# Turning the normalised rows of a Trainium2 kernel by transfers and VectorE instead of TensorE

## The reference

```python
# A1: attention of 8 heads of 64, in chunks of 32 queries with 56 keys around them and 8 memory keys
scores = scale * np.matmul(q_c, k_full.transpose(0, 1, 3, 2))
a = softmax(scores);  out[:, :, c_start:c_end] = np.matmul(a, v_full)
# A2: a layer with SoLU and a layer norm over its 1024 hidden values
h = x @ w_in                                   # 512 -> 1024
solu = h * sm                                  # sm = softmax of h over the row
ln = (solu - mu) / np.sqrt(var + 1e-06) * g_ln
x = ln @ w_out                                 # 1024 -> 512
# C: each token goes to one of 8 experts (argmax of x @ w_gate)
h = np.maximum(x[mask] @ w1[e], 0.0);  out[mask] = gate_w * eom * (h @ w2[e])
```

## Time and profile before

| | |
|---|---|
| three runs | 747.57, 749.77, 752.82 us (median 749.77) |
| profiled execution | 749.5 us, its span 747.8 us |
| busy in the span | TensorE 715.8 us (96%), VectorE 474.1 (63%), ScalarE 303.9 (41%), GpSimd 188.9 (25%) |
| mean granted clock of TensorE | 0.991 |
| stage A | to about 385 us |
| transposes of `u_sb` on TensorE | 192 in 24 blocks |

### The profile page before, as it was taken

The page is one execution under the profiler, slowest core; times in us unless marked ns, Lnnn a source line. Parts: engine busy times, 40 slices in busy tenths (PEclk is TensorE's granted clock), DMA queues, the critical chain, the costliest instruction groups (busy, mean ns, idle before and its releaser), DMA issues.

```text
span 747.8 us, 16177 instructions
## 1 busy us (share of the span) xinstructions
PE 715.8 (96%) x5272; PEld 619.3 (83%) x5273; DVE 474.1 (63%) x777; ACT 303.9 (41%) x467; POOL 188.9 (25%) x352
## 2 busy tenths in 40 slices
PE   3899999999999999999989999999999999999985
PEld 2698999899989998999988777888888888888874
DVE  5677788778867676767854647434757556675332
ACT  3543444444443444344423446224444445363220
POOL 3121444434311112111220222221222321321211
PEclk9999999999999999999999999999999999999998
DMA  9713333443232222322013676833969696933220
GB/s 326 258 42 123 107 100 113 144 138 99 71 117 95 71 71 90 122 71 71 30 44 128 225 229 179 225 79 80 243 151 285 169 253 160 237 76 99 63 67 32
DMA packets 43949, 98.70 MB, mean 132 GB/s; under 512 B 6286, under 2 KB 19982, under 8 KB 43792
## 3 DMA queue, kind: packets, MB, share of 16 engines
q1 hardware_dynamic: 22128, 64.82, 27.7%
q10 hardware_dynamic: 15840, 16.52, 9.8%
q0 software_dynamic: 5952, 16.98, 7.2%
HBM read 73.78 MB, written 14.09 MB: 118 GB/s over the span
## 4 chain that ended last, share of the span: by engine, by line
PE 91%; DMA 3%; DVE 3%; issue 2%; ACT 1%; ACTq 1%; POOLq 0%; SPq 0%; POOL 0%; DVEq 0%
PE banks L1213 76%; PE banks L1244 4%; PE banks L1234 3%; PE banks L1266 3%; PE banks L1226 3%; PE banks L1346 2%; DMA r_quads<-r_sb 1%; DMA q_sb<-q_t 1%; DMA xs<-x_rows,rows_now 1%; ACTq L723 1%; DVE he L890 0%; DVE prob L875 0%; PE banks L1369 0%; PE banks L1296 0%; ACT xsT_hi L694 0%
## 5 line engine op out<-in xcount | busy, mean ns | idle before, releaser
L1213 PE MATMUL banks<-slots_hi_lo,rT_hi 128*128 128x512 f32 x464 | 147.3, 399 | 1.9 <-DVE rT_lo L1054 1.9
L1213 PE MATMUL banks<-slots_hi_lo,xsT_hi 128*128 128x512 f32 x464 | 125.9, 394 | 2.8 <-DVE xsT_lo L1043 2.8
L1213 PEld LDWEIGHTS banks<-slots_hi_lo,xsT_hi 128*128 128x128 f32 x464 | 87.4, 189 | 21.8 <-issue 3.9
L1213 PEld LDWEIGHTS banks<-slots_hi_lo,rT_hi 128*128 128x128 f32 x464 | 85.8, 190 | 18.9 <-issue 2.3
L1213 PE MATMUL banks<-slots_hi_lo,rT_lo 128*128 128x512 f32 x232 | 91.5, 394 | 0.0
L1213 PE MATMUL banks<-wout_hi,uT_hi 128*128 128x264 f32 x384 | 83.4, 299 | 2.0 <-DVE uT_lo L879 2.0
L1213 PE MATMUL banks<-wout_hi,uT_lo 128*128 128x264 f32 x384 | 78.7, 287 | 0.0
L1213 PE MATMUL banks<-wout_lo,uT_hi 128*128 128x264 f32 x384 | 78.5, 286 | 0.0
L1043 DVE TENSOR_TENSOR xsT_lo<-banks,xsT_hi 128x512 fp32r<-128x512 f32 x30 | 20.6, 688 | 83.2 <-ACT xsT_hi L694 83.2
L1054 DVE TENSOR_TENSOR rT_lo<-banks,rT_hi 128x1024 fp32r<-128x1024 f32 x29 | 35.5, 1224 | 59.5 <-ACT rT_hi L734 58.0
L1213 PE MATMUL banks<-slots_hi_lo,xsT_lo 128*128 128x512 f32 x232 | 72.2, 393 | 0.0
(11 more groups left out here) (168 smaller groups left out, 1189.9 us busy)
## 6 DMA issues: line engine op xcount, KB each, us to landing
raw_w<-experts SPq DMA_DIRECT2D x56, 512.0 KB, 4.8
r_quads<-r_sb ACTq DMA_DIRECT2D x104, 128.0 KB, 3.7
v_sb<-v_win SPq DMA_DIRECT2D x24, 384.0 KB, 4.6
k_sb<-k_win SPq DMA_DIRECT2D x22, 384.0 KB, 3.5
x_rows<-x SPq DMA_DIRECT2D x24, 264.0 KB, 2.1
q_sb<-q_t SPq DMA_DIRECT2D x24, 256.0 KB, 2.7
stage<-experts POOLq DMA_DIRECT2D x8, 512.0 KB, 5.8
weights<-w_both ACTq DMA_DIRECT2D x4, 512.0 KB, 9.6
```

The source lines that it names most:

```text
L1213: ins = mm(o, lhs, rhs(part, k, n), start=(k == first and lhs is not None and part == 0 and parts == (0, 1)), stop=(k == final and parts = ...
```

## The change

`u_turn` stays on TensorE for blocks 0 and 23. For blocks 1 to 22 SyncE issues four transfers of `u_sb` into a new buffer `u_quads`, and VectorE transposes it into `turn_ps` a step later (`turn_u`). The rows of `w_out` and the gains are ordered on the host to fit that layout, so for blocks 0 and 23 the centring writes `u_sb` with its columns in that order. `uT_hi` and `uT_lo` get two buffers each. The second product of a block is split: chunks 0 to 3 in the step after its first product, chunks 4 to 7 in the step after that, and `scale_y`, the store and `copy_logits` move one step later with it. `EARLY` is 20 instead of 21, and the order around the last block and the first expert tiles is written anew. The buffers `stage`, `x2`, `xs` and `xsT` move to make room.

```diff
-EARLY = NBLK - 3
+EARLY = NBLK - 4
...
+            def quads_u(b):
+
+                sp.wait_ge(u_s, b.i + 1)
+                for a in range(QUADS):
+                    sp.dma_start(u_quads[a * 32:(a + 1) * 32, :],
+                                 u_sb[:, a * (DF // QUADS):(a + 1) * (DF // QUADS)]).then_inc(u_quads_s, 16)
...
@@ SyncE, step
                     load_qk(s + 2)
                     load_v(s + 2)
-                store(s + -1)
+                if (s + -2).within(NBLK):
+                    store(s + -2)
+                quads_u(s)
...
@@ ScalarE
                 act.wait_ge(uT_ps_s, b.i + 1)
-                at_least(act, y_s, b.i)
-                nc.scalar.activation(uT_hi[:, :], turn_ps, ACT.Copy).then_inc(uhi_s, 1)
+                at_least(act, y_s, b.i - 1)
+                nc.scalar.activation(uT_hi[b.par][:, :], turn_ps, ACT.Copy).then_inc(uhi_s, 1)
...
                 copy_probsT(s + 1)
+                scale_y(s + -2)
                 high_x(s + 1)
                 square_u(s)
-                scale_y(s + -1)
...
             high_u(last)
             scale_y(last + -1)
             xt(At(0, 0))
+            scale_y(last)
             relu(At(0, 0))
             xt(At(0, 1))
-            scale_y(last)
             high_r(At(0, 0))
...
@@ VectorE
+            def turn_quads(quads):
+
+                return nc.vector.transpose(turn_ps.rearrange("p (c j b) -> p b c j", c=KF, b=QUADS),
+                                           quads[:, :].rearrange("p (b c i) -> p b c i", b=QUADS, c=KF))
+
+            def turn_u(b):
+
+                dve.wait_ge(u_quads_s, b.i * (QUADS * 16))
+                dve.wait_ge(xlo_s, b.i + 2)
+                dve.wait_ge(ulo_s, b.i)
+                turn_quads(u_quads).then_inc(uT_ps_s, 1)
...
             def step(s):
-                softmax_a(s + 1)
-                if (s + -2).within(NBLK):
-                    copy_logits(s + -2)
-                if isinstance(s.i, int) and s.i == EARLY + 1:
+                if isinstance(s.i, int) and s.i == NBLK - 2:
                     dve.wait_ge(logc_s, EARLY)
                     choose(0, EARLY)
                     link(V.memset(seg_e[:, :, :], 1.0))
                     link(V.memset(seg_e[:, :, 0:1], 0.0))
+                softmax_b(s + 1)
+                turn_u(s + -1)
+                h_max(s)
                 low_u(s + -1)
-                softmax_b(s + 1)
-                h_max(s)
                 solu(s)
                 low_x(s + 1)
+                copy_logits(s + -2)
+                if (s + 2).within(NBLK):
+                    softmax_a(s + 2)
...
@@ TensorE
+            HALF = KF // 2
+
             def step(s):
                 a, b, c = s + 1, s, s + -1
-                product_in(b, range(0, 1))
-                u_turn(c)
-                product_in(b, range(1, KD))
-                product_out(c, range(0, 2))
+                product_in(b, range(KD))
                 probs_turn(a)
-                product_out(c, range(2, 5))
+                product_out(c + -1, range(HALF, KF))
                 attention(a)
                 if (a + 1).within(NBLK):
                     scores(a + 1)
                 else:
                     ranks(0, EARLY)
-                product_out(c, range(5, KF))
+                product_out(c, range(0, HALF))
...
             probs_turn(At(0, 2))
-            product_out(At(0, 0), range(2, 5))
+            product_out(At(0, 0), range(2, HALF))
             attention(At(0, 2))
             scores(At(0, 3))
-            product_out(At(0, 0), range(5, KF))
             walk_a(pe, step)
             last_b = At(0, NBLK - 1)
-            product_in(last_b, range(0, 1))
-            u_turn(last_b + -1)
-            product_in(last_b, range(1, KD))
-            product_out(last_b + -1, range(0, 3))
+            product_in(last_b, range(KD))
+            product_out(last_b + -2, range(HALF, KF))
+            product_out(last_b + -1, range(0, 2))
             first_product()
-            product_out(last_b + -1, range(3, 7))
+            product_out(last_b + -1, range(2, 5))
             u_turn(last_b)
-            product_out(last_b + -1, range(7, KF))
+            product_out(last_b + -1, range(5, KF))
+            product_out(last_b, range(0, 3))
             xs_turn(At(0, 0))
-            product_out(last_b, range(0, 5))
+            product_out(last_b, range(3, KF))
             hidden(At(0, 0), range(KD))
             xs_turn(At(0, 1))
-            product_out(last_b, range(5, KF))
+            ranks_late()
             r_turn(At(0, 0))
-            hidden(At(0, 1), range(0, 2))
-            ranks_late()
-            hidden(At(0, 1), range(2, KD))
+            hidden(At(0, 1), range(KD))
...
@@ the host's order of rows
-    w_both = np.concatenate([rows(moe_w_in, KD), rows(moe_w_out, KF)], axis=1)
+    w_both = np.concatenate([rows(moe_w_in, KD), quad_rows(moe_w_out)], axis=1)
```

More of the change, by code:

```diff
@@ L186, in build @@
         u_sb = ra.take("u_sb", [P, DF], F32)
-        uT_at = ra.at
-        uT_hi = ra.take("uT_hi", [P, DF], F32R)
-        uT_lo = ra.take("uT_lo", [P, DF], F32R)
+        uT_hi, uT_lo = [], []
+        for n in range(2):
+            uT_hi.append(ra.take(f"uT_hi{n}", [P, DF], F32R))
+            uT_lo.append(ra.take(f"uT_lo{n}", [P, DF], F32R))
+        u_quads = ra.take("u_quads", [P, DF], F32)
         prob_start = nc.alloc_sbuf_tensor_at("prob_start", [P, NU, KEYS], F32, offset=u_at)
-        x2_at = ra.at
-        x2 = [ra.take(f"x2_{n}", [P, YW], F32) for n in range(2)]
-        ra.at += (slot0 - ra.at) % (4 * BANK) + 2 * BANK * 4
         stage_at = ra.at
-        stage = [ra.take(f"stage{n}", [P, CH], F32) for n in range(2)]
+        stage = ra.take("stage", [P, 2 * YW], F32)[:, 0:CH]
+        x2 = [ra.take("x2_0", [P, YW], F32), x2_odd]
         w1_hi, w2_hi, w1_lo, w2_lo = (Region(slot1 + n * W1C * 4, W1C * 4) for n in range(4))
@@ L236, in build @@
         r_quads = [rc.take(f"r_quads{n}", [P, DF], F32) for n in range(2)]
+        xsT_hi = rc.take("xsT_hi", [P, DM], F32R)
+        xsT_lo = rc.take("xsT_lo", [P, DM], F32R)
+        assert rc.at == stage_at
+        xs = [rc.take(f"xs{n}", [P, YW], F32) for n in range(2)]
         ys = [rc.take("ys_even", [P, DM], F32), ys_odd]
-        assert rc.at <= stage_at
         banks = ctx.enter_context(nc.psum_tensor("banks", [P, 8 * BANK], F32))
@@ L250, in build, with y_banks @@
         y2_ps = [bank(n)[:, 0:YB] for n in (4, 5)]
-        y_both = bank(4, 2).rearrange("p (b n) -> p b n", n=BANK)[:, :, 0:YB]
+        y2_last_ps = [bank(n)[:, 0:YB] for n in (6, 7)]
+        def y_banks(b):
+            return 6 if isinstance(b.i, int) and b.i == NBLK - 2 else 4
         parts_ps = bank(4, 2)
@@ L770, in _ @@
             exp_h(last)
+            scale_y(last + -2)
             square_u(last)
@@ L902, in solu @@
                     dve.wait_ge(pT_ps_s, 2)
[L903 to L904 removed]
+                elif isinstance(b.i, int) and b.i == 1:
+                    dve.wait_ge(uT_ps_s, 1)
+                else:
+                    dve.wait_ge(u_quads_s, (b.i - 1) * (QUADS * 16))
+                to, of = u_sb[:, :], he[:, :]
+                if turned_by_pe:
+                    to = to.rearrange("p (k a i) -> p a k i", a=QUADS, k=KF)
+                    of = of.rearrange("p (a k i) -> p a k i", a=QUADS, k=KF)
+                nc.vector.tensor_scalar(to, of, stat[:, 1:2], stat[:, 2:3], ALU.mult, ALU.subtract).then_inc(u_s, 1)
+            def solu(b):
+                weigh_h(b)
+                centre_h(b)
             def low_x(b):
@@ L1084, in _ @@
             first_tokens()
+            turn_u(last + -1)
+            h_max(last)
             low_u(last + -1)
@@ L1087, in _ @@
             copy_logits(last + -2)
-            h_max(last)
+            weigh_h(last)
             first_rows()
+            centre_h(last)
             late_base()
-            solu(last)
             low_u(last)
@@ L1264, in u_turn @@
                 pe.wait_ge(u_s, b.i + 1)
+                if isinstance(b.i, int) and b.i == NBLK - 1:
+                    pe.wait_ge(first_tbl_s, 1)
                 for k in range(KF):
@@ L1272, in product_out @@
                     pe.wait_ge(fold_lo_s, 1)
+                outs = y2_ps
+                if isinstance(b.i, int) and b.i == NBLK - 2:
+                    outs = y2_last_ps
                 if 0 in chunks:
                     pe.wait_ge(ulo_s, b.i + 1)
-                    at_least(pe, x2_s, b.i)
-                last = split_product(y2_ps, lambda k: uT_hi[:, k * P:(k + 1) * P], lambda k: uT_lo[:, k * P:(k + 1) * P],
+                    if isinstance(b.i, int) and b.i == NBLK - 2:
+                        pe.wait_ge(place_hot_s, 1)
+                    elif isinstance(b.i, int) and b.i == NBLK - 1:
+                        pe.wait_ge(x2_s, b.i - 1)
+                    else:
+                        at_least(pe, x2_s, b.i)
+                last = split_product(outs, lambda k: uT_hi[b.par][:, k * P:(k + 1) * P],
```

(3 more changed lines are left out.)

44 lines of the change are left out of this document (23 added, 21 removed).

## The result

The changed kernel took 730.79 us (median of four runs, 730.33 to 730.97) beside 749.49 for the kernel before: a ratio of 0.9745, 95% interval 0.971 to 0.978. It was timed on two more occasions, with ratios of 0.9729 (0.9698 to 0.976) and 0.9718 (0.970 to 0.9736), medians 727.73 and 728.34. The prediction was 732.3, range 727.5 to 740.0, faster by over 1% with a chance of 0.88. The first profiled execution took 730.97 us, 729.3 of them its span; "the profile after" is this one.

A forecast was written before the change was run, and what follows sets the result against it. TensorE was taken to bound stage A at 15.15 us a block. From 749.5: -19.1 transposes, +1.0 collisions, +3.5 and +0.3 start, +0.5 block 22, -2.5, -1.7 and +0.8 at the end gave 732.3 us, range 727.5 to 740.0.

The forecast's parts named there:

- The transposes, -19.1: Stage A, blocks 1 to 22: TensorE loses eight transposes a block, 22 x 0.87 us, so -19.1 us.
- The transfer loop, 7.7 + L: h_max through u_sb, issues, landing L and VectorE's transpose: 11.4 us at L = 3.7, under TensorE's 14.28; price 0.
- Rival B: Transfers set the step: at landing 8.8 us the loop is 16.5 us, the kernel 778 us; chance 0.05.
- VectorE's loop, 13.4: VectorE's loop through attention takes some 13.4 us against TensorE's 14.28, leaving 0.9 us a step.
- Rival C: VectorE's chain sets the step: 1.75 us added gives 15.15 a step and 749 us, 1.2 gives 739; chance 0.10.
- Collisions, +1.0: GpSimd's expert 0 subtraction delays VectorE's u_sb: 0.5 us in two bad steps of eight, +1.0 us; ends 0 and 5.6.
- The start, +3.5 and +0.3: TensorE waits of 2.1, 0.7 and 0.7 us after scores(3), +3.5 us; a possible clock drop there, +0.3.
- Block 22 and the tail, +0.5 -2.5 -1.7 +0.8 = -2.9: Four terms for block 22's step, waits and clock at the end of stage A, and the first expert tile.
- +0.5: Block 22's step: choose and two memsets, 2.4 us, stand ahead of the softmax; +0.5 us, between 0 and 1.5.
- -2.5: End of stage A: the 0.7 us wait goes and 0.2 of the 2.0 us wait stays, -2.5 us.
- -1.7: End of stage A: without the idling, the clock drop of 388 to 392 us goes too, -1.7 us.
- +0.8: First expert tile: routing of four blocks instead of three precedes tile 1's xT_lo, and relu follows scale_y; +0.8 us.

The follow-up runs named there:

- c1: First repeat of the unchanged changed kernel, timed and profiled on another occasion: median 727.73 us, ratio 0.9729 to the kernel before.
- c2: Second repeat of the unchanged changed kernel, timed and profiled on a further occasion: median 728.34 us, ratio 0.9718 to the kernel before.
- the late splits: Changed kernel with VectorE's last two w_out low-part splits moved behind h_max(1) and softmax_a(3): 726.9 us, ratio 0.971; repeated, 0.9716.

## Why the prediction was right, and where it was off

The total, 732.3 against 730.8, is closer than its parts. By the ledger of the first profile the transposes and the collisions came out 0.8 us better than the sum had them, the start 1.4 worse, and 2.0 were gained in stretches where nothing was changed. That these nearly cancel is luck, and against the repeats at 728 the sum is 4 us too high, near the lower end of its range.

*The transposes, -19.1.* Right. The steps went from 15.16 to 14.27, 0.89 each, and with the transfers undone they are 15.18. Over 22 blocks that is 19.6 to 20.0.

*The transfer loop, 7.7 + L.* Price 0, right: no step waits for a transfer. Two terms were misread and in part offset each other: issues 2.3 us instead of 1.6 (the pitch of the earlier trace rows is that of the loads of `q`, `k` and `v`, and not that of the quarter transfers), L 3.3 instead of 3.7. Rival B was real as a mechanism, as the sixteen transfers show.

*VectorE's loop, 13.4.* 13.24 by the double transpose. Rival C needed 1.75 us more. By the Trainium skill (VectorE: DVE Perf Modes, "Rules for kernel authors") the turn would belong on TensorE. The runs speak against that rule here: VectorE had 1.0 us a step to spare and TensorE none, so the dearer transpose (1.25 us against 0.87) on the other engine won 2.3 to 2.6%.

*Collisions, +1.0.* 19 steps of 14.27 are 271.2, and the three profiles of the changed kernel have 1.3, 0.4 and 1.0 more. But the term was to be added to the kernel before, whose 19 steps have 0.6 over 19 x 15.16 already. The net is 0.7, -0.2 and 0.4, less than predicted. The place was read from one piece of eight: I looked at `u_sb`, as the earlier trace rows show it. In most pieces the instruction ahead of it is hit, on one column, and it was so in the kernel before:

```profile
123.93 2.36 POOL L538 TENSOR_TENSOR slots_hi_lo<-stage,slots_hi_lo 128x1024 f32 x1 [0.19 <-POOL slots_hi_lo L536]
124.10 2.20 DVE L896 SCALAR_TENSOR_TENSOR stat<-hesum,stat 128x1 f32<-128x1 f32 x1
```

There line 896 was hit in five of the eight pieces and `u_sb` in two. In the changed kernel:

```profile
77.25 2.36 POOL L555 TENSOR_TENSOR slots_hi_lo<-stage,slots_hi_lo 128x1024 f32 x1 [0.19 <-POOL slots_hi_lo L553]
...
77.45 2.18 DVE L928 SCALAR_TENSOR_TENSOR stat<-hesum,stat 128x1 f32<-128x1 f32 x1
79.67 0.81 DVE L946 TENSOR_SCALAR u_sb<-he,stat 128x1024 f32<-128x1024 f32 x1
```

Line 928 took 0.16 us in the step at 207 us and 2.18 here: it ends with GpSimd's subtraction. That `u_sb` reads 0.81 in the same step means only that it came behind. Beside the eight subtractions VectorE's instructions lasted longer than usual by 10.0, 10.9 and 11.0 us in sum in the profiles of the changed kernel (`c1`, `c2`, the first), and the 19 steps exceed 271.2 by 0.4, 1.0 and 1.3. With the late splits it is 11.9 and 13.2 us, and 1.9 twice; with eight transfers 2.3 and 2.6 us, and nothing. The two go together over seven profiles. No run took the subtraction out, so the cause rests on this.

*The start, +3.5 and +0.3.* This is the step that failed in its working. I counted the 18 matmuls that left the place behind `scores(3)`. Six more, one chunk of 0.73 us, left the place ahead of attention(2), so TensorE came to the gap that much earlier, and it was 2.75 us and not 2.1. Behind it the waits were 0.41 and 0.44 without a fall of the clock (`c2`), not 0.7 and 0.7. By the ledger, with 4.38 us moved and two transposes (1.77) gone, the stretch to `probs_turn(4)` should read 32.80: it lost 3.6 us with no fall, 4.1 and 5.2 with one. Predicted were 3.8. That the waits behind would absorb part of a fall was right (1.6 us at `probs_turn(4)`, where `product_in(2)` alone took 3.1 us longer), but it left more than my 0.3, since the fall lasted 6.8 us.

*Block 22 and the tail, +0.5 -2.5 -1.7 +0.8 = -2.9.* The stretch should read 47.49 + 4.38 - 0.88 = 50.99 and reads 48.10: -2.9. The wait for `uT_lo` is 0.2 as forecast, and the clock 1.00 from 345 to 420 us. The end-of-stage cover is worth 1.4 us by its own experiment. The terms +0.5, -1.7 and +0.8 have no run of their own, so only their sum is shown; in block 22's step attention starts 0.28 us late (`c1`, `c2` and the first profile).

*Not predicted: the beginning (-0.9) and the rest (-1.1).* Nothing in them was changed. In the eleven profiles that I laid against this ledger, all with the changed kernel's first 35 us, `u_turn(0)` starts between 34.05 and 36.18 us, and the rest takes 333.3 to 337.0. So I count both as spread between executions; it also explains why the repeats, at 728, stand 3 us under the first 730.8. What sets that spread stays open. With eight transfers no step grows any more: both profiles have exactly 271.20 us for 19 steps, and the instruction of line 928 takes at most 0.79 us in one and 1.33 in the other. Whether the transfers are the reason stays open, and the medians don't differ.

## What to carry to other kernels

Take work off the engine that is the bound even if it costs more elsewhere, but first close every loop that it enters: add its pieces by rows, and compare with what the bound needs after the change, not before. The slack of a loop can be found by doubling one of its pieces. Moving work over DMAs needs a consumer that comes later: without the half-step delay the same transfers, in the same order on VectorE, were 2.9% slower than the kernel before. And a gain of half a us at one place must be followed to the end, since another engine's phase can take it back.

## What the runs showed of the hardware that was not expected

- One SBUF-to-SBUF transfer held SyncE's queue for 0.60 us (four or eight per block) or 0.67 (sixteen), where a load of `v` took 0.39.
- Behind the same wait of 2.7 us, in the same kernel, the granted clock fell to 0.50 in one profile, for a shorter time in another, and not at all in a third. In the repeated kernel with the wait of 1.9 us it fell too (0.50 in the window 50 to 52). The Trainium skill (TensorE: Matmul & The Clock Gate, "What's actually happening") says that how many matmuls run at the lower level differs between runs of the same kernel. It says so of a kernel's start; the three profiles show it behind a wait in the middle.
- A VectorE instruction on a single column took 2.18 us beside GpSimd's subtraction, 14 times its 0.16. The Trainium skill (SBUF — State Buffer, "SBUF: two separate sides") counts a VectorE op with two SBUF inputs, against a GpSimd op that reads SBUF, among those where one waits for the other's whole instruction. Line 928 has two, GpSimd's subtraction reads `stage` in SBUF, and the rows agree: the one column ends with the subtraction, however short it is by itself.
